# The experts' two products woven together in one kernel on one core: each up product between down products, two steps ahead

## What is computed

```
for t in range(S):
    state = alpha[:, :, t, :, None] * state + einsum('bhd,bhe->bhde', k[:, :, t], v[:, :, t])
    y[:, :, t] = einsum('bhd,bhde->bhe', q[:, :, t], state)
x = y as (3072 tokens, 384)
x = ((x @ w1) * (x @ w2) @ w3) @ w_out            # 384 -> 1024 -> 1024 -> 384
p = domain_probs / (domain_probs.sum(-1) + 1e-9)
for e in range(4):
    h = maximum(x @ moe2_w1[e], 0)                # 384 -> 1024, the up product
    out += p[:, e:e + 1] * (h @ moe2_w2[e])       # 1024 -> 384, the down product
```

## Time and profile before

| | us |
|---|---|
| median of 3 runs | 1232.59 |
| lowest and highest | 1231.42, 1234.31 |
| profiled execution, its own time | 1234.97 |
| its span, first to last instruction | 1233.2 |

### The profile page before, as it was taken

One profiled execution on the slowest core, in us unless ns is written; L12 is line 12 of the kernel. 1 busy time (PEld: TensorE's weight loads), 2 busy tenths in 40 slices (PEclk: granted clock), 3 DMA queues, 4 the chain that ended last, 5 costly groups with the idle time before them and its releaser, 6 DMA issues.

```text
span 1233.2 us, 18720 instructions
## 1 busy us (share of the span) xinstructions
PE 1223.9 (99%) x7714; PEld 1113.7 (90%) x7714; DVE 441.3 (36%) x873; ACT 276.7 (22%) x515; POOL 168.2 (14%) x148
## 2 busy tenths in 40 slices
PE   9999999999999999999999999999999999999999
PEld 5699999999999999999899998999989999999898
DVE  4876765765751122222222222221222222222222
ACT  1433333333332411111111111111111111111111
POOL 1122222222222630000000000000000000000000
PEclk9998999999999999999999999999999999999999
DMA  9634645644622440111141111113011111222200
GB/s 276 211 78 102 144 101 123 140 104 123 144 56 109 142 169 25 50 51 52 52 154 52 52 51 51 52 52 134 24 49 51 52 52 52 78 77 77 77 19 33
DMA packets 81638, 107.49 MB, mean 87 GB/s; under 512 B 36000, under 2 KB 54688, under 8 KB 81056
## 3 DMA queue, kind: packets, MB, share of 16 engines
q1 hardware_dynamic: 81568, 106.50, 29.1%
HBM read 86.03 MB, written 18.09 MB: 84 GB/s over the span
## 4 chain that ended last, share of the span: by engine, by line
PE 92%; DVE 3%; DMA 2%; SPq 1%; issue 0%; ACT 0%; DVEq 0%; ACTq 0%
PE bank L938 26%; PE bank L940 26%; PE bank L939 25%; PE score_banks L938 3%; PE score_banks L939 3%; PE score_banks L940 3%; PE bank L1121 2%; DMA keys_t<-keys_spill 1%; PE bank L1136 1%; PE bank L977 1%; PE bank L987 1%; PE score_banks L998 1%; PE score_banks L963 1%; DMA keys_spill<-key_blocks 1%; SPq L318 1%; SPq L310 1%
## 5 line engine op out<-in xcount | busy, mean ns | idle before, releaser
L762 DVE SCALAR_TENSOR_TENSOR h_lo<-bank,h_hi 128x512 fp32r<-128x512 f32 x192 | 132.9, 692 | 617.4 <-ACT h_hi L556 617.4
L556 ACT ACTIVATE h_hi<-bank 128x512 fp32r<-128x512 f32 x192 | 115.1, 600 | 663.6 <-PE bank L940 663.6
L940 PE MATMUL bank<-x_hi,we_lo 128*128 128x512 f32 x576 | 228.3, 396 | 0.0
L939 PE MATMUL bank<-x_lo,we_hi 128*128 128x512 f32 x576 | 227.3, 395 | 0.0
L938 PE MATMUL bank<-x_hi,we_hi 128*128 128x512 f32 x576 | 226.6, 393 | 0.0
L939 PE MATMUL bank<-we_lo,h_hi 128*128 128x384 f32 x576 | 192.6, 334 | 0.0
L940 PE MATMUL bank<-we_hi,h_lo 128*128 128x384 f32 x576 | 192.6, 334 | 0.0
L938 PE MATMUL bank<-we_hi,h_hi 128*128 128x384 f32 x576 | 192.6, 334 | 0.0
L459 POOL TENSOR_TENSOR we_lo<-we_raw,we_hi (+1 forms) x48 | 60.9, 1291 | 529.4 <-ACT we_hi L517 529.4
L940 PEld LDWEIGHTS bank<-x_hi,we_lo 128*128 128x128 f32 x576 | 108.4, 188 | 24.8
L938 PE MATMUL bank<-x,wb_hi 128*128 128x384 f32 x384 | 129.0, 336 | 1.3 <-DVE g_sb L752 1.3
(11 more groups left out here) (89 smaller groups left out, 1436.7 us busy)
## 6 DMA issues: line engine op xcount, KB each, us to landing
x_hi<-x_hi_spill SPq DMA_DIRECT2D x24, 768.0 KB, 4.9
x_lo<-x_lo_spill SPq DMA_DIRECT2D x24, 768.0 KB, 6.4
inputs<-akq SPq DMA_DIRECT2D x24, 672.0 KB, 5.5
we_raw<-wset SPq DMA_DIRECT2D x4, 3072.0 KB, 10.2
values<-v_rows SPq DMA_DIRECT2D x24, 256.0 KB, 5.8
x_hi_spill<-x_hi_out SPq DMA_DIRECT2D x8, 576.0 KB, 3.4
x_lo_spill<-x_lo_out SPq DMA_DIRECT2D x8, 576.0 KB, 4.4
keys_spill<-key_blocks SPq DMA_DIRECT2D x60, 64.0 KB, 1.8
```

The costliest lines, as they stand in the source:

```text
L556: act.activation(h_hi[:, s % 2, :], bank[s % 2][:, :], ACT.Relu).then_inc(h_hi_ready, 1)
L762: dve.scalar_tensor_tensor(out=h_lo[:, s % 2, :], in0=bank[s % 2][:, :], scalar=0.0, in1=h_hi[:, s % 2, :], op0=ALU.max, op1=ALU.subtract) ...
L939: pe.matmul(dst, left[0], right[1], start=False, stop=False)
L940: return pe.matmul(dst, left[1], right[0], start=False, stop=last)
```

## The change

`up2` is taken apart into `up2_waits` and `up2_product`, which issues one of the nine products, and `down2` into `down2_product`, one of the twelve. `step2` issues the twelve down products of step s, and behind each whose number isn't a multiple of four one of the nine up products of step s + 2. So the order within a step is D D U D U D U three times over, with D a down product of 384 columns and U an up product of 512. Steps 0 and 1 of the first expert have their up products ahead of it, in blocks of nine as before; the last two steps of the last expert have no up products beside them. The wait for `a_ready` is written in front of the calls instead of in `up2`. The waits, signals, banks and buffers are the same, and all other engines' programs too.

```diff
--- before.py
+++ after.py
@@ -63,6 +63,8 @@
 FOLD_FIRST = 5
 FOLD_BANKS = [0, 1, 2, 3, 4, 0, 1, 2]
 SUM_BANKS = [5, 2, 3, 4]
+TERMS = 3
+assert KT * TERMS == SUBS * TERMS - TERMS
 WARM = 6
 CONSTANTS = 7
 FLAG_STEP = STEPS1 - 4
@@ -1072,19 +1074,27 @@
                 if f == FT - 1:
                     mm.then_inc(x1_done, 1)
 
-            def up2(e, m, s):
+            def up2_waits(e, m, s):
                 u, f = divmod(s, FT)
-                if isinstance(m, int) and (e, m, s) == (0, 0, 0):
-                    pe.wait_ge(a_ready, STEPS1 * BATCH)
                 if f == 0:
                     pe.wait_ge(x1_loaded[u], 32 * (e * ROUNDS + m + 1))
                     if u == 0 and isinstance(m, int) and m == 0:
                         pe.wait_ge(piece_lo, PIECES * (e + 2))
-                for k in range(KT):
-                    cols = slice(k * FF + f * P, k * FF + (f + 1) * P)
-                    mm = split_product(bank[s % 2][:, :], (we_hi[e % 2][:, cols], we_lo[e % 2][:, cols]),
-                                       (x1_hi[u][:, k, :], x1_lo[u][:, k, :]), k == 0, k == KT - 1)
-                mm.then_inc(up_done, 1)
+
+            def up2_product(e, s, i):
+
+                u, f = divmod(s, FT)
+                k, term = divmod(i, TERMS)
+                cols = slice(k * FF + f * P, k * FF + (f + 1) * P)
+                mm = pe.matmul(bank[s % 2][:, :], (we_hi if term < 2 else we_lo)[e % 2][:, cols], (x1_lo if term == 1 else x1_hi)[u][:, k, :],
+                               start=(i == 0), stop=(i == KT * TERMS - 1))
+                if i == KT * TERMS - 1:
+                    mm.then_inc(up_done, 1)
+
+            def up2(e, m, s):
+                up2_waits(e, m, s)
+                for i in range(KT * TERMS):
+                    up2_product(e, s, i)
 
             def bilinear(b, beside=True, last_batch=False):
                 for s in range(STEPS1):
@@ -1101,6 +1111,7 @@
                         over_redo = pe.mark_branch_hint_location()
                     if last_batch and beside and s == STEPS1 - 1:
                         with pe.If(flag == 1):
+                            pe.wait_ge(a_ready, STEPS1 * BATCH)
                             up2(0, 0, 0)
                     down1(b, s)
                     if last_batch and beside and s == FT - 1:
@@ -1168,35 +1179,48 @@
                     up1(BATCH + b, 0, 0, False)
                     up1(BATCH + b, 0, 1, False)
                     bilinear(BATCH + b, beside=False)
+                pe.wait_ge(a_ready, STEPS1 * BATCH)
                 up2(0, 0, 0)
                 pe.addr_align(256, max_nops=0)
                 pe.br("experts")
             nc.switch_bb("experts")
 
-            def down2(e, m, s):
+            def down2_product(e, m, s, i):
+
                 u, f = divmod(s, FT)
+                sub, term = divmod(i, TERMS)
+                if term == 0 and e == 0 and s == 0 and sub >= 1:
+                    pe.wait_ge(x1_lo_ready, X1_LOW_AHEAD + KT * (TILES1 * BATCH - 1) + sub)
+                if term == 0 and f == 0:
+                    pe.wait_ge(added, SUBS * (e * TILES2 + 2 * m + u) + sub + 1)
+                rows = slice(sub * P, (sub + 1) * P)
+                cols = slice(KT * FF + f * DM, KT * FF + (f + 1) * DM)
+                mm = pe.matmul(bank[SUM_BANKS[sub]][:, 0:DM], (h_hi if term < 2 else h_lo)[:, s % 2, rows], (we_lo if term == 1 else we_hi)[e % 2][:, cols],
+                               start=(f == 0 and term == 0), stop=(f == FT - 1 and term == TERMS - 1))
+                if f == FT - 1 and term == TERMS - 1:
+                    mm.then_inc(down_done, 1)
+
+            def step2(e, m, s, ahead):
+
                 pe.wait_ge(h_lo_ready, STEPS2 * (e * ROUNDS + m) + s + 1)
-                cols = slice(KT * FF + f * DM, KT * FF + (f + 1) * DM)
-                for i in range(SUBS):
-                    if e == 0 and s == 0 and i >= 1:
-                        pe.wait_ge(x1_lo_ready, X1_LOW_AHEAD + KT * (TILES1 * BATCH - 1) + i)
-                    if f == 0:
-                        pe.wait_ge(added, SUBS * (e * TILES2 + 2 * m + u) + i + 1)
-                    rows = slice(i * P, (i + 1) * P)
-                    mm = split_product(bank[SUM_BANKS[i]][:, 0:DM], (h_hi[:, s % 2, rows], h_lo[:, s % 2, rows]),
-                                       (we_hi[e % 2][:, cols], we_lo[e % 2][:, cols]), f == 0, f == FT - 1)
-                    if f == FT - 1:
-                        mm.then_inc(down_done, 1)
+                if ahead:
+                    up2_waits(*ahead)
+                ups = 0
+                for i in range(SUBS * TERMS):
+                    down2_product(e, m, s, i)
+                    if ahead and i % SUBS >= 1:
+                        up2_product(ahead[0], ahead[2], ups)
+                        ups += 1
 
             def round2(e, m, following):
 
                 for s in range(STEPS2):
-                    if s + 1 < STEPS2:
-                        up2(e, m, s + 1)
-                    elif following:
-                        up2(*following, 0)
-                    down2(e, m, s)
-
+                    if s + 2 < STEPS2:
+                        step2(e, m, s, (e, m, s + 2))
+                    else:
+                        step2(e, m, s, following and (*following, s + 2 - STEPS2))
+
+            up2(0, 0, 1)
             for e in range(EXPERTS):
                 with pe.Fori(0, ROUNDS - 1) as m:
                     round2(e, m, (e, m + 1))
```

## The result

| | before | after |
|---|---|---|
| median, us | 1232.67 | 1230.38 |
| ratio to before, 95% interval | | 0.9983 [0.9975, 0.9991] |
| profiled execution | 1234.97 | 1231.72 |
| its span | 1233.2 | 1230.0 |

Each median is over 22 executions; one of each kernel fell far outside (3110.46 and 1713.53 us) and is left out of the ratio. The changed kernel is faster by about 2.3 us. The forecast was 10.7 us off, to 1222, with a range of 1219 to 1230.

What follows compares the result with a forecast made beforehand. PE, busy for 1223.9 of 1233.2 us, was taken to bound the kernel by its products' spacing. 11.6 + 1.1 - 2.0 = 10.7 us off the median of 1232.6 gave 1222 us, with a range of 1219 to 1230.

Steps and rivals of the forecast that it cites:

- The change of bank: At nearly every product of the experts' stage PE goes to another bank; claimed to cost zero for 384 columns.
- The sign: Whether the whole kernel gets faster or slower; faster was claimed, by 10.7 us, at a chance of 0.82.
- Something that builds up over neighbouring 512 column products makes each later one dearer.: In the experts' blocks of nine U, each later U was claimed to cost 4 to 9 ns more.
- the full gain: In the experts' stage, the saving of U and D together if no extra stays: 12.7 us.
- The U term: In the experts' stage, each U between D costs what a block's first costs now: 11.6 us off.
- The D term: In the experts' stage, three D behind each block lose an extra 2 ns each over 190 steps: 1.1 us off.
- What stays: The part of the extra left in the woven experts' steps: between nothing and 8.0 us, taken as 2.0 us.
- the high bound: Most extra left in the experts' steps: six U a step pay 4 ns, nine D 2 ns; 8.0 us.
- the after-effect: In the experts' stage, neighbouring U make later U 4 to 9 ns dearer and the next D 2 ns.
- Slower: Rival, chance 0.09: in the experts' stage U to D is dear, U 234.5 ns, D 175; 7.2 us more, 1239.8 us.
- Partial, 1228 to 1231: Rival, chance 0.04: in the experts' stage the extra goes by how many U stand among the last few products.
- No change: Rival, chance 0.09: in the experts' stage spacing follows a product's own columns and accumulation, not neighbours; 1232.6 us.

Runs made afterwards that it cites:

- e3_blocks_ahead: The changed kernel with its lead of two steps, but nine U in one block behind the twelve D; step 4.173 us, ratio to before 1.0007.
- e2_mixtures: Kernel before plus sixteen streams of 384 and 512 column mixtures, other banks, fixed moving data or low weights behind its end; a pair of D and U took 406.7 ns.
- e13_aligned_after: The changed kernel with three unused tiles that start every operand at a multiple of 512 bytes; step 4240.0 ns, ratio to before 1.0083.
- the grid: Kernel before plus steps in both orders behind its end, h and x shifted over 8 x 8 places; means 4188.2 ns (order before) and 4190.3 ns (woven).
- e7_lone: The changed kernel with the step order six D, one U, six D, eight U; step 4220.0 ns, 1242.56 us in one execution.
- e8_places: Kernel before plus seventeen streams of 40 products with fixed weights of varied place and value; 512 columns took 226.7 to 234.2 ns.
- e11_shifts: Kernel before plus twenty streams of 40 products, weights and moving data shifted against each other; 512 columns took 226.7 ns at 0 and 256 bytes, 233.4 at 32.
- e15_placed_after: The changed kernel with three unused tiles of 128, 192 and 192 bytes a partition; step 4120.0 ns, median 1222.87 us, ratio to before 0.992.
- e5_alternate: The changed kernel with the step order D D D, then D U nine times; step 4200.0 ns, 1238.05 us, ratio to before 1.005.
- e1_sizes: Kernel before plus eleven streams of 48 products of different widths, with 128 or 64 weight columns; 233.4 ns at 512 columns, 173.4 at 384.
- e4_feed: Kernel before plus seven streams of 48 products with zero moving data, zero weights or bf16 copies; at 512 columns 233.4, 226.7 and 215.84 ns.
- e6_threes: The changed kernel with the step order D D D D U U U three times; mean step 4200.0 ns, 1239.28 us, ratio to before 1.0059.
- e16_placed_before: Kernel before with unused tiles of 224, 64 and 224 bytes; steps of 4142 and 4205 ns by turns, 4173.3 on average, ratio to before 1.0005.

## Why the prediction was right and wrong

**Right: what bounds the kernel, and that no wait matters.** PE is full at a clock of 1.00 and has no wait beyond the first stage; h_lo, the additions, the weights of the next expert and x1 came in time. e3_blocks_ahead shows the lead at 1.0007 [0.9994, 1.0021]. The change of bank costs nothing, for 512 columns as well (233.4 against 233.4 ns, e2_mixtures), which only 384 columns in the earlier trace rows had shown. The sign was right too, but by luck: the reason given for it was not the cause, the same weaving costs 53 ns a step at the places of e13_aligned_after, and over the grid it is the longer order as often as the shorter.

**Wrong: "Something that builds up over neighbouring 512 column products makes each later one dearer."** This is the step that failed, and the size with it. The rows showed four facts (a cheap first U, a dearer second, dear later ones, a short tail in the D), and I read one cause into them. A lone U does cost about 226 ns, in the change and in e7_lone, but not because it is alone: the third U of each seven stands between two D and costs 232.5, and in the stream of pairs every U does. The D pay a part of what the U save, and in e7_lone, at up to 185.0 ns, more than all of it. The streams give 226.7 or 233.4 for the same 512 columns beside the same neighbours by the place of the weights alone (e8_places, e11_shifts).

**Wrong in size: the full gain.** The U term was 11.6 us and brought 6.7. The D term was 1.1 us off and came as 4.1 us on. It was too large from the start: the three D behind a block stood only 0.9, 0.9 and 1.7 ns above the others before, 3.5 ns a step and not 6, since a ns of modelled duration isn't a ns of spacing there. "384 column products stand 173 ns apart wherever they are" is the sentence that fell: they stand at 172.5 to 180.0 in the change.

**Wrong: the bound of "What stays".** Of the 12.7 us, 2.5 came, so 10.2 stayed, above the high bound of 8.0. That bound let a U pay what the second of a block pays and a D what it pays behind nine, and so took the after-effect for granted in its own worst case. The median, 1230.4, lies just outside the range, which ends at 1230.

**The rivals.** "Slower" was argued away with a stall at the step from U to D, seen in one row behind eight U and explained by them. Its 175 ns for a D came true on average (2105.0 / 12 = 175.4), and so did one of its signs, 384 column products of over 336 ns (338). Its threshold, a pair of U and D at over 0.406 us, did not decide: the stream of pairs shows 0.4067, and the changed kernel is faster all the same. With the aligned places (e13_aligned_after) the woven order is slower, at 4.240 us a step. The forecast's step of 4.11 to 4.13 us came in the end too, at 4.120, with e15_placed_after. So both outcomes exist with this order, and what chooses between them, the place of the tiles, was named by none of the cases.

"Partial, 1228 to 1231" has the measured time in it, at a chance of 0.04. Its cause, the number of 512 column products among the last few, isn't the one either: with the same order e15_placed_after and e13_aligned_after take 4120 and 4240 ns a step, and e5_alternate, with no two U side by side, takes 4200. The number came in by luck.

"No change" rested on the start flag of the first product. The changed trace clears it: the first U of the second and the third seven have no start flag and take the same 226.6 ns as the first U of all.

**The rule.** The Trainium skill, "TensorE: Matmul & The Clock Gate", section "Back-to-back issue gap", has N/2.4 + 2.5 ns for an isolated product at the full clock. In bf16 the streams follow it: 215.84 ns at 512 columns, 162.5 at 384 and 109.2 at 256, all within 0.1 ns. The kernel's 32-bit products don't: in the streams they take 226.7 at best and 233.4 at the kernel's places.

## What to carry to other kernels

Where PE is full with 32-bit products, a difference of some ns between places in a repeating order is no evidence on neighbours: measure the step as a whole, and try the tiles' places (some 32 bytes of unused columns) before and beside the order, since the same order went from 4120 to 4240 ns a step by them alone (e15_placed_after, e13_aligned_after). When rows show a pattern with several parts, ask of each cause which part it would forbid, and bound the sum by the loss as well as by the gain. A short bench behind the kernel names the effect, but its number counts only once the whole kernel has shown it.

## What the runs showed of the hardware

- In streams of 512 column products with fp32r operands, the spacing is 226.7 to 234.2 ns by the distance between the weights and the moving operand modulo 256 bytes (e8_places, e11_shifts). Neither value (e8_places), bank nor the part of the weights (e2_mixtures) moves it.
- From 128 to 512 columns the spacing of fp32r products follows about 3 ns + 0.447 ns a column with 64 columns of weights ((231.6 - 60.0) / 384 = 0.447, e1_sizes), where bf16 follows 0.417 from 256 to 512 ((215.84 - 109.2) / 256, e4_feed).
- With a load of 128 columns of weights for each, fp32r products stand no closer than 111.6 ns, with 64 columns of weights 60.0 or less (e1_sizes).
- The steps repeat to within 2 ns over some 190 repetitions (by pairs in e6_threes and e16_placed_before), and in every kernel their mean length was a multiple of 6.67 ns to within 0.2 ns (4120, 4160, 4173.3, 4186.7, 4200, 4220, 4240).
